# Early activation-table load and a respaced first block in a gated-scan and ELU feed-forward kernel

## The reference

```python
sig = 1.0 / (1.0 + np.exp(-f_logit))
f = lower_bound[None, None, :] + (1.0 - lower_bound[None, None, :]) * sig
i = 1.0 - f
for t in range(S):
    h = f[:, t] * h + i[:, t] * x[:, t]
    y[:, t] = h
...
h = x @ w_in
g = np.where(h > 0.0, h, alpha * (np.exp(np.minimum(h, 0.0)) - 1.0))
return (g @ w_out).astype(np.float32)
```

## Time and profile before

| | |
|---|---|
| median of three runs | 961.97 us |
| the profiled execution | 961.75 us |
| its span, from first to last instruction | 959.9 us |
| PE busy | 954.5 us (99%) |
| ScalarE busy | 790.1 us |
| VectorE busy | 722.9 us |
| GpSimd busy | 628.8 us |
| instructions | 15015 |

### The profile page before, as it was taken

The page is one execution under the profiler, slowest core; times in us unless marked ns, Lnnn a source line. Parts: engine busy times, 40 slices in busy tenths (PEclk is TensorE's granted clock), DMA queues, the critical chain, the costliest instruction groups (busy, mean ns, idle before and its releaser), DMA issues.

```text
span 959.9 us, 15015 instructions
## 1 busy us (share of the span) xinstructions
PE 954.5 (99%) x4362; PEld 815.6 (85%) x4362; DVE 722.9 (75%) x916; ACT 790.1 (82%) x1424; POOL 628.8 (66%) x475
## 2 busy tenths in 40 slices
PE   9999999999999999999999999999999999999998
PEld 6999888888888888888888888888888888888887
DVE  6998976976886796697688679678768867966444
ACT  7989888878888888888888888888888788887775
POOL 2588796576667668557656755856775765676544
PEclk9999999999999999999999999999999999999999
DMA  7212012002102201100210210120021021001001
GB/s 273 68 33 95 1 33 66 34 1 78 55 1 57 76 1 44 55 33 2 74 55 0 66 66 0 46 66 18 23 65 44 0 76 55 0 0 46 1 1 45
DMA packets 23078, 42.02 MB, mean 44 GB/s; under 512 B 2560, under 2 KB 4096, under 8 KB 23040
## 3 DMA queue, kind: packets, MB, share of 16 engines
q1 hardware_dynamic: 22752, 41.10, 13.2%
q10 hardware_dynamic: 288, 0.46, 0.2%
HBM read 29.10 MB, written 12.45 MB: 43 GB/s over the span
## 4 chain that ended last, share of the span: by engine, by line
PE 95%; ACT 2%; DVE 1%; issue 0%; DMA 0%; ACTq 0%; DVEq 0%
PE acc L893 17%; PE acc L895 17%; PE acc L894 17%; PE h L863 14%; PE h L865 14%; PE h L864 14%; ACT e L469 1%; PE h L998 1%; PE h L1000 1%; PE h L999 1%; ACT e L463 1%; DMA opening<-first_gate 0%; DVE x L625 0%; ACT opening L419 0%; PE h L964 0%
## 5 line engine op out<-in xcount | busy, mean ns | idle before, releaser
L335 POOL TENSOR_TENSOR g_lo<-e,g_hi 128x512 fp32r<-128x512 f32 (+1 forms) x384 | 516.6, 1356 | 325.2 <-ACT g_hi L477 323.8
L463 ACT ACTIVATE e<-h 128x512 f32<-128x512 f32 (+1 forms) x379 | 224.9, 594 | 124.3 <-PE h L865 90.1
L716 DVE SCALAR_TENSOR_TENSOR e<-e,h 128x512 f32<-128x512 f32 (+1 forms) x379 | 256.8, 677 | 70.2 <-ACT e L469 69.0
L893 PE MATMUL acc<-g_hi,w_out_hi 128*128 128x512 f32 (+1 forms) x768 | 291.1, 379 | 0.4 <-DVE w_out_lo L687 0.4
L895 PE MATMUL acc<-g_hi,w_out_lo 128*128 128x512 f32 (+1 forms) x768 | 291.0, 379 | 0.0
L894 PE MATMUL acc<-g_lo,w_out_hi 128*128 128x512 f32 (+1 forms) x768 | 290.9, 379 | 0.0
L469 ACT ACTIVATE e<-e 128x512 f32<-128x512 f32 (+1 forms) x384 | 241.2, 628 | 9.6 <-issue 1.1
L477 ACT CAST g_hi<-e 128x512 fp32r<-128x512 f32 (+1 forms) x384 | 232.0, 604 | 19.4 <-DVE e L716 19.4
L863 PE MATMUL h<-a_hi,w_in_hi 128*128 128x512 f32 x616 | 234.7, 381 | 0.0
L865 PE MATMUL h<-a_hi,w_in_lo 128*128 128x512 f32 x616 | 234.7, 381 | 0.0
L864 PE MATMUL h<-a_lo,w_in_hi 128*128 128x512 f32 x616 | 234.7, 381 | 0.0
(11 more groups left out here) (75 smaller groups left out, 555.8 us busy)
## 6 DMA issues: line engine op xcount, KB each, us to landing
opening<-forget_logit SPq DMA_DIRECT2D x44, 256.0 KB, 2.6
x<-value SPq DMA_DIRECT2D x44, 256.0 KB, 2.7
out<-out_sb SPq DMA_DIRECT2D x44, 256.0 KB, 2.0
w_in_raw<-w_in SPq DMA_DIRECT2D x8, 256.0 KB, 5.5
w_out_raw<-w_out SPq DMA_DIRECT2D x8, 256.0 KB, 6.6
out<-out_sb SPq DMA_DIRECT2D x4, 224.0 KB, 2.1
x<-value SPq DMA_DIRECT2D x3, 224.0 KB, 6.3
opening<-forget_logit SPq DMA_DIRECT2D x2, 224.0 KB, 6.4
```

Of the source, the lines that this page charges most:

```text
L335: nc.gpsimd.tensor_tensor(g_lo[:, t % RING, 0:w], e[:, t % TILES, 0:w], g_hi[:, t % RING, 0:w].bitcast(F32), ALU.subtract).then_inc(g_lo_r ...
L463: nc.scalar.activation(e[:, i, 0:w], bank_of(j, t)[:, 0:w], ACT.Relu, scale=-1.0).then_inc(r_ready, 1)
L716: nc.vector.scalar_tensor_tensor(e[:, t % TILES, 0:w], e[:, t % TILES, 0:w], -1.0, bank_of(j, t)[:, 0:w], ALU.add, ALU.max).then_inc(g_rea ...
L893: nc.tensor.matmul(bank, hi, g_h, start=opens, stop=False)
```

## The change

It has two parts. In the head, ScalarE first waits for VectorE's `carry` and GpSimd's zero tile, loads its activation table for a one-column tanh into `p5`, and only then starts its two transfers; SyncE's list is the same as before. The warm-up has 14 matmuls in place of 18. In the first block the hand-written tables are respaced: as a rule one extra operation a tile, and of the eight pairs' weight sums only the first four are made in block 0; the sums of pairs 4 to 7, their rounding and their rests go to block 1, through new `second_spare` functions of ScalarE and VectorE. The special handling of the last pair's first sum (`round_last_sum`) goes away.

```diff
-WARM_UP = 18
+WARM_UP = 14
...
+            act.wait_ge(warm_ready, 1)
+            act.wait_ge(coef_ready, 1)
+            nc.scalar.activation(p5[:, 0:1], e[:, 0, 0:1], ACT.Tanh, bias=carry[:, 0, 0])
             act.dma_start(gate[:, 0, 1, 0:SHORT], forget_logit[0, :, 1, tokens(0)]).then_inc(gate_loaded[0][1], 16)
             act.dma_start(x[:, 0, 1, 0:SHORT], value[0, :, 1, tokens(0)]).then_inc(x_loaded[0][1], 16)
...
             def first_spare(t):
-                if t in (0, 2, 3, 6, 13):
-                    round_plain({0: 3, 2: 4, 3: 5, 6: 6, 13: 7}[t])
-                if t in (1, 4, 7, 8, 10, 12, 18):
-                    round_w_out({1: 1, 4: 2, 7: 3, 8: 4, 10: 5, 12: 6, 18: 7}[t])
+                if t in (0, 2, 3, 6, 14):
+                    round_plain({0: 3, 2: 4, 3: 5, 6: 6, 14: 7}[t])
+                if t in (1, 4, 7, 8, 10, 11, 24):
+                    round_w_out({1: 1, 4: 2, 7: 3, 8: 4, 10: 5, 11: 6, 24: 7}[t])
...
-                if t == 30:
-                    for p in range(PAIRS // 2, PAIRS - 1):
-                        round_sums(p)
-                    round_sums(PAIRS - 1, P6)
...
+            def second_spare(q):
+
+                if q in (2, 3, 4, 5):
+                    round_sums(q + 2)
...
-                if t in (16, 18, 20, 24):
-                    w_sum(PAIRS // 2, PAIRS // 2, {16: 0, 18: 1, 20: 2, 24: 3}[t])
...
+            def second_spare(q, place):
+
+                if place == 3 and q in (0, 1):
+                    w_sum(PAIRS // 2, PAIRS // 2, 2 * q)
+                    w_sum(PAIRS // 2, PAIRS // 2, 2 * q + 1)
```

## The result

The changed kernel takes 1001.94 us (median of five, 998.97 to 1003.35) against 961.55 us (median of five) before: ratio 1.0408, 95% interval 1.0389 to 1.0426. It is slower by 40 us where 1.8 us of gain were forecast. The profiled execution took 1002.26 us with a span of 1000.4 us.

A forecast was written before the change was run, and what follows sets the result against it. PE bounds the kernel, gapless from block 1 on. From the profiled 961.75 us, block 0 -1.7 and block 1, head and warm-up 0 give 960.05; with 0.22 for the median 960.27, stated as 960.2, range 959.0 to 962.6.

The forecast's parts named there:

- Block 0: -1.7: Block 0: respacing moves the causes of four late PE starts; 1.7 of 1.87 us gone, ends 0.9 and 1.87.
- Head: 0: Head: earlier first gate and later ScalarE transfers offset; between -0.35 and +0.4 us, taken as 0.
- my lower bound: Head: ScalarE's transfers start at 1.27 us if the queue runs ahead of the table load; 2.4 was taken.
- my upper bound: Head: the first gate, without its companion transfer, gains between 0 and 1.3 us; 0.45 was taken.
- rival A: Head: ScalarE's transfers start later than 2.4 us, second gate at 7.5, loss 1.4 us; 961.7 us, chance 0.13.
- Warm-up: 0: Head: four warm-up matmuls fewer only shorten filler ahead of 8.47 us; no cost or gain unless the clock reacts.
- rival B: Warm-up: with 14 matmuls the clock may rise too late, real matmuls run at 0.373 us; 963 us, chance 0.09.
- Work moved to block 1: 0, or its overhang once: Block 1: sums, casts and rests moved there cost nothing; without cover, the overhang once, since later pairs shift with PE.
- 3.3 us of cover: Block 1: pair 4's weights are ready near 113.2 us, PE needs them about 116.5.
- The time is the moment at which block 1 begins plus a constant.: Whole kernel: from 79.50 to 950 us PE runs gapless at 0.22 us, so only earlier starts before that gain.
- a few matmuls spaced a little wider than normal: Block 0: these follow each of four late starts, so each costs more than its gap; counted in 1.87 us.
- Rival D: Head and block 0: the head gains fully (0.35 us or more) and all 1.87 us goes; 959.6 us, chance 0.12.

The follow-up runs named there:

- e1: The changed kernel with 18 warm-up matmuls again instead of 14, all else as changed: 1002.35 us, ratio 1.0415.
- e2: The kernel before with only the change's head and 14 warm-up matmuls: ratio 0.9996; seven of eleven executions 961.4 to 962.2 us, four 1004.1 to 1005.2.
- n2: The kernel before with one extra VectorE maximum over 1792 weights in block 2, pair 4, at about 200 us: 998.88 us, ratio 1.0390.
- run 278: Not a follow-up run: "run" is a verb here, and 278 ns is the first gap listed behind the late start of 66.55.
- r2: The changed kernel with 24 extra matmuls of 448 columns at the start of block 2: 967.26 us, ratio 1.0077.
- d1: The changed kernel with 10 extra matmuls of 448 columns at the start of block 1: 1002.05 us, ratio 1.0418.
- c2: The changed kernel with block 1's four VectorE weight sums spread and the next block's first gate opened one place later: 1000.62 us, ratio 1.0394.
- n11: The kernel before with one extra VectorE maximum over 1792 weights in the last block, pair 2: 961.47 us, ratio 0.9999.
- r1: The changed kernel with 12 extra matmuls of 256 columns at the start of block 2: 999.58 us.

## Why the prediction was wrong

- **Block 0: -1.7, in truth -1.86.** Right; all four late starts went, and no new one came there.
- **Head: 0, in truth 0.** Right in sum by luck, wrong in its parts. The queue ran ahead of the table load, my lower bound, and not in order. The first gate gained 1.3 us, my upper bound, not 0.45. Both gains ended at the second input, which I had not followed. The drain after the load, rival A, was not there: the small tanh began at 2.26, with the load over at 2.24.
- **Warm-up: 0.** Right as far as is seen (e1 with 18 loses the same 40 us, e2 with 14 none in its undisturbed executions), and rival B did not show.
- **Work moved to block 1: 0, or its overhang once. This step failed.** There were two errors in it. I had looked at the dates at which PE wants weights, with 3.3 us of cover, and they were indeed never late. I had not looked at the short chains that go once a product through VectorE, whose slack was some tenths of a us: one more or one slower instruction ahead of L710 or L702 used it up. And GpSimd's placement was costed by busy shares and by when its own results were due, though it sets how long VectorE's instructions take (0.68 or 1.50 us), a spread that the prediction itself had noted for the sums.
- **"The time is the moment at which block 1 begins plus a constant."** This sentence failed most. It held PE's gap of 0.22 us for a property of the matmul. n2 shows that it is a property of the stream, which one late start can change; in the profiled execution of the changed kernel the turn behind a start 22 ns late cost 42 us, where the sum had 0. The sign of it stood in the trace of the kernel before: behind the late start of 66.55 the gaps run 278, 207, 216, 207, 199, 215, 199, 195 ns before they are at 193 again. The prediction saw them, "a few matmuls spaced a little wider than normal", and counted them in block 0's 1.87 us, but did not ask what they would do where nothing narrower than 512 columns follows. A wait in the gapless part was named as what could lose, and then priced at its own length.
- **The chances** gave 0.03 to slower. The sign was excluded by a sum of known waits, with no room for a rate that changes. (Rival D's own terms, 961.97 less 0.35 less 1.87, give 959.75 and not 959.6; nothing hangs on it.)

## What to carry to other kernels

In a long gapless stream of weight loads and matmuls, count matmuls in equal windows and read start-to-start gaps, not the busy share: 456 against 436 in 100 us stood beside 99% busy in both. Where such a stream has an undisturbed rhythm, its worth is the gain times all that follows, so slack ahead of each of its waits comes before a shorter prologue. A row of 24 matmuls a little narrower brought the rhythm back in r2, after 11 of them; fewer were not tried on purpose, and the six that block 1 has by itself were enough in two profiles and not in others. Work moved off a crowded stretch is costed by the tightest wait near its new place and by what it does to the engine it shares memory ports with, not by average idle time.

## What the runs showed of the hardware

- 512-column matmuls, each with its own weight load, keep to 220.0 ns or to 230.7 ns start to start, with the same program, operands and granted clock; 448-column ones to 193.3 or 200.0; with operands read in plain order 226.7. The Trainium skill (TensorE: Matmul & The Clock Gate, "Back-to-back issue gap") gives about 131 ns at 512 columns for a sustained stream of loads and matmuls, and N / 2.4 + 2.5 ns for an isolated matmul's gap, by which an estimate is 215.8 ns. None of the three rhythms is either, and the page has one value for a stream at each width, not two; the measured ones decide here.
- In the undisturbed rhythm the matmul starts 29 to 31 ns after its load ends, in the other one 36 to 47. A load that began only 42 or 70 ns after the previous matmul, done 6 ns before its own matmul began or 29 ns after, was enough for the turn (d1, c2); one of 35 ns, done 12 ns before, healed after six wide gaps (c2), and one of 395 ns turned nothing (r2, 888.03). Of twelve late starts that met the undisturbed rhythm among 512-column matmuls only, in all profiles, ten turned it and two did not. No profile shows a turn to the slower rhythm without a late start at its place. What in the engine holds the lateness, and what decides between the two outcomes, is not settled.
- 256-column matmuls with their loads follow each other at 111 to 120 ns while each load lasts 187 ns, so loads overlap and a load's length is no floor of the spacing; and 12 of them do not restore the rhythm, while 24 of 448 columns do.
- At 448 columns most late starts of block 0 healed within 1 to 15 matmuls or met the next late start on the way. Three did not: in n2 and n11 the gaps stayed at 199 and 201 for some 70 matmuls, until the next late start, and in e2 to the end of block 0. At 512 columns the slower rhythm, once it had lasted some 20 matmuls, ended by itself in no profile; it ended at 448-column matmuls (r2) and at late starts in the last block, near 922 us (r1 and d1), where in other profiles (after, e1) a late start at the same matmul left it as it was.
